# A Fourier filter with routed experts: the 128-point transforms split by a radix-2 step into four tiles of the matrix engine

## The chip, the cores and the metric

One core of one Trainium2 chip runs the kernel. It has five engines with a queue of instructions each: TensorE (PE: matmuls; PEld: its weight loads), VectorE (DVE), ScalarE (ACT), GpSimd (POOL) and SyncE (SP), which only issues transfers; ACT and POOL issue transfers too (rows with a q, as ACTq). An engine works through its own queue in order and waits on semaphores for the others. The time is the device time of one execution in microseconds, the median of the runs.

## The reference

The input x has 8 batches of 3072 rows with 256 features. Each feature is filtered along the rows in the frequency domain, and the result goes through a layer of experts that takes every row at most once.

```python
X = np.fft.rfft(x, axis=1)
Y = X * (filt_r + 1j * filt_i)[None, :, :]
x = np.fft.irfft(Y, n=3072, axis=1).reshape(24576, 256)

logits = x @ w_gate                      # 8 experts, softmax, the largest one is taken
# expert e keeps the first 768 rows that chose it, in order of the rows
h = np.maximum(np.einsum('ecd,edf->ecf', disp, w1), 0.0)   # 768 rows, 1024 wide
y = np.einsum('ecf,efd->ecd', h, w2)
# a kept row becomes gate * y, every other row of the output is zero
```

Since an expert keeps only its first 768 rows, the kernel transforms three batches (FIRST = 3), looks whether every expert is full, and transforms the other five only where one is not. In the runs here three were enough.

## The kernel before

**The transform.** 3072 is split as 128 times 24 (N1 = 128, N2 = 24): row 24*n1 + n2. The steps for batch t are these.

1. `x_load` brings x in six chunks of four n2 (x_in, 128 partitions by n1). `pe_a` multiplies each half chunk by the 128x128 matrix wa, a 128-point Fourier transform over n1 that gives 64 real and imaginary pairs ("units"), into one of two PSUM banks; `act_a` copies it on ScalarE to t_out (three buffers for six chunks; for batch 0 the last three go to v_in) and stores it to DRAM (zt, the profile's t_scratch), two stores a chunk: the even partitions, then the odd ones. Batch 0 goes through this alone; later batches within the stage of the batch before (stage 0 from its step 8, else from step 0, in four steps, A_STEPS).
2. Stage t: `z_load` brings zt back in eight groups, with frequencies of n2 on partitions. In each of 16 steps h `pe_forward` makes eight 64x64 tile matmuls into the PSUM tile wide, VectorE multiplies by the filter (pq, line 599), and in every even step from 2 on, and once after the last, `pe_inverse` makes the inverse transform over n2 of two earlier steps into back; `act_back` copies to v_out and stores to DRAM (vt, u_scratch).
3. Tokens of batch t, within the next stage: `v_load` brings six chunks into v_in (three buffers, each waiting until the matmuls of the chunk three earlier are done), `pe_product` multiplies by the 128x128 matrix wai, `act_rows` copies to y and `act_rows_out` stores the rows (y_rows); `pe_turn` transposes with the identity, `pe_logits` and `pe_raw` make the expert scores. `pe_tokens` and `act_tokens` call them by a step i from 0 to AI_SPAN-1: product i, turn i-1, logits and raw behind. They start at step h = AI_FROM = 4, in the last stage at AI_EARLY = 3, and what is left over runs on in the next stage.
4. Routing of a batch: 30 short VectorE steps (`dve_route`) from the scores to the list of tokens, in the last stage a few per step h (STEPS_BY) behind each pq, later in `dve_last`. Two small matmuls (`pe_rank`, at step ai_from + RANK_STEP) and one set of 24 (`pe_table`) belong to it.

The last batch's tokens have no stage after them: `sp_last`, `pe_last`, `act_last`, `dve_last` and `pool_last` run them alone, beside the routing of batch 1 and the first expert weights (`raw_load` on SP, `act_split` and `low_split`).

**Constants.** wf, wbi and fab (the filter) come in four table groups: group 0 by SP at the start, the others by POOL once batch 0's stores have landed, with batch 1's x between them. Before that fab and wbi are zeroed, by VectorE (wbi, fab's first quarter) and POOL (the rest).

**The experts** follow: 16 blocks of 384 gathered rows, products in two float32 parts, rows scattered to the output. Their code isn't touched.

## Time and profile before

| | |
|---|---|
| time, median of 3 runs | 573.71 us (572.97 to 573.96) |
| the profiled execution: time, span of its instructions | 571.98 us, 570.1 us |
| mean granted TensorE clock | 0.944 of full speed |
| TensorE matmul busy | 483.7 us (85%) |
| VectorE, ScalarE, POOL busy | 220.1, 213.7, 216.8 us |
| moved by DMA | 121.22 MB, mean 213 GB/s |

The span runs from the first to the last instruction. Busy shares are averages over parts of unlike kind: transforms until about 248 us, experts after it. Times in the rows below are microseconds from the start of the span; names in front of an arrow are what an instruction writes.

### The profile page before, as it was taken

What the parts mean: (1) busy time and instruction counts of PE and PEld (TensorE: products, weight loads), DVE (VectorE), ACT (ScalarE), POOL (GpSimd) and SP (SyncE); (2) the same over time, 40 slices, a digit from 0 to 9 for tenths busy, and PEclk for the clock granted to TensorE, in tenths of its full rate; (3) what the DMA queues carried; (4) which work ended last, traced back from release to release, by engine and by line L of the source; (5) the groups of instructions that cost most, each with busy time, mean ns of one, the idle gap of its engine ahead of it and who ended that gap; (6) DMA issues with size and microseconds to landing.
All of it is one profiled execution on the core that took longest, in us unless ns stands there. A gap on an engine that the chain in (4) does not pass through costs nothing.

```text
span 570.1 us, 9642 instructions
## 1 busy us (share of the span) xinstructions
PE 483.7 (85%) x3864; PEld 386.9 (68%) x3864; DVE 220.1 (39%) x334; ACT 213.7 (37%) x378; POOL 216.8 (38%) x189
## 2 busy tenths in 40 slices
PE   5457676899989958977981699999999999999995
PEld 2124232355545534667971699999999999999994
DVE  6024132233355769167700453324433244332210
ACT  2202222444525535635110445424454244443320
POOL 7070100000000000484077227765587655876212
PEclk9859998999989988899986799999999999999999
DMA  8899997979677649789721021983119741193001
GB/s 293 304 348 414 411 309 242 324 246 288 209 243 263 214 133 341 275 291 407 255 83 55 18 93 43 384 296 113 46 62 388 279 129 37 57 389 129 28 21 43
DMA packets 63973, 121.22 MB, mean 213 GB/s; under 512 B 7696, under 2 KB 35120, under 8 KB 63920
## 3 DMA queue, kind: packets, MB, share of 16 engines
q1 hardware_dynamic: 37824, 66.17, 33.4%
q10 hardware_dynamic: 16304, 29.01, 14.3%
q0 software_dynamic: 9792, 25.34, 12.4%
q8 instruction: 33, 0.54, 0.4%
q14 instruction: 20, 0.16, 0.1%
HBM read 60.69 MB, written 59.81 MB: 211 GB/s over the span
## 4 chain that ended last, share of the span: by engine, by line
PE 73%; DMA 8%; issue 5%; DVE 5%; ACT 4%; ACTq 3%; SPq 0%; POOLq 0%; POOL 0%; DVEq 0%
PE back L1050 22%; PE wide L1036 12%; PE bank L1036 12%; PE back L364 7%; PE bank L390 6%; PE wide L351 4%; PE bank L379 3%; DMA v_in<-u_scratch 3%; DMA t_scratch<-t_out 2%; PE bank L403 2%; ACTq L505 2%; DVE pq L599 2%; PE bank L1019 2%; PE bank L417 1%; ACT t_out L498 1%
## 5 line engine op out<-in xcount | busy, mean ns | idle before, releaser
L1050 PE MATMUL back<-w2h,hh 128*128 128x256 f32 x384 | 110.4, 288 | 1.0 <-ACT o_out L823 1.0
L1050 PE MATMUL back<-w2l,hh 128*128 128x256 f32 x384 | 109.3, 285 | 0.0
L1050 PE MATMUL back<-w2h,hl 128*128 128x256 f32 x384 | 109.3, 285 | 0.0
L599 DVE TENSOR_TENSOR pq<-wide,fab 128x1024 f32<-128x1024 f32 x48 | 58.8, 1224 | 118.2 <-PE wide L351 118.2
L865 DVE SCALAR_TENSOR_TENSOR hl<-wide,hh 128x384 fp32r<-128x384 f32 x64 | 34.6, 555 | 133.8 <-ACT hh L814 104.8
L954 POOL DMA_INDIRECT out<-o_out,token x48 | 52.3, 1090 | 82.2 <-ACT o_out L823 72.6
L1050 PEld LDWEIGHTS back<-w2h,hh 128*128 128x128 f32 x384 | 74.3, 194 | 1.2 <-ACT o_out L823 1.2
L1050 PEld LDWEIGHTS back<-w2h,hl 128*128 128x128 f32 x384 | 74.4, 194 | 0.0
L1050 PEld LDWEIGHTS back<-w2l,hh 128*128 128x128 f32 x384 | 74.3, 194 | 0.0
L926 POOL DMA_INDIRECT g_in<-y_rows,token x48 | 51.4, 1072 | 57.2 <-DVE token L737 35.1
L823 ACT ACTIVATE o_out<-back,o_gate 128x256 f32<-128x256 f32 x48 | 22.7, 476 | 103.4 <-PE back L1050 86.5
L1036 PE MATMUL wide<-xh,w1h 128*128 128x384 f32 x128 | 44.6, 349 | 18.9 <-issue 17.0
L379 PE MATMUL bank<-x_in,wa 128*128 128x512 f32 x72 | 40.4, 683 | 18.3 <-ACT t_out L498 11.9
L938 POOL DMA_INDIRECT o_gate<-gate_rows,token x48 | 48.7, 1014 | 14.6 <-issue 14.6
L917 POOL DMA_DIRECT2D gate_rows<-gate x3 | 1.7, 569 | 134.7 <-DVE gate L672 93.8
L364 PE MATMUL back<-pq,wbi 64*48 64x256 f32 x768 | 51.0, 407 | 2.0 <-DVE pq L599 2.0
L351 PE MATMUL wide<-z_in,wf 64*64 64x256 f32 x384 | 33.0, 414 | 21.6 <-DMA z_in<-t_scratch 11.7
L512 ACT COPY v_out<-back 112x1024 f32<-112x1024 f32 x24 | 24.3, 1013 | 59.9 <-PE back L364 53.6
L865 DVE SCALAR_TENSOR_TENSOR hl<-bank,hh 128x384 fp32r<-128x384 f32 x64 | 35.0, 555 | 29.4 <-ACT hh L814 22.4
L390 PE MATMUL bank<-v_in,wai 128*128 128x512 f32 x72 | 41.9, 668 | 4.7 <-DMA v_in<-u_scratch 3.8
L814 ACT ACTIVATE hh<-wide 128x384 fp32r<-128x384 f32 x64 | 30.4, 492 | 40.3 <-PE wide L1036 18.5
L1036 PE MATMUL bank<-xh,w1h 128*128 128x384 f32 x128 | 43.6, 340 | 1.9 <-DVE hl L865 1.9
(109 smaller groups left out, 802.8 us busy)
## 6 DMA issues: line engine op xcount, KB each, us to landing
out<-zero SPq DMA_DIRECT2D x24, 1024.0 KB
w_raw<-in_w SPq DMA_DIRECT2D x16, 1024.0 KB
u_scratch<-v_out ACTq DMA_DIRECT2D x48, 192.0 KB, 3.6
v_in<-u_scratch SPq DMA_DIRECT2D x36, 256.0 KB, 5.2
y_rows<-y ACTq DMA_DIRECT2D x18, 512.0 KB, 3.8
t_scratch<-t_out ACTq DMA_DIRECT2D x30, 256.0 KB, 6.2
z_in<-t_scratch SPq DMA_DIRECT2D x24, 256.0 KB, 3.8
x_in<-in_x POOLq DMA_DIRECT2D x12, 512.0 KB, 15.3
```

The source lines that it names most:

```text
L351: mm = nc.tensor.matmul(wide[out_half, a, 0, :], wf[half, 2 * h + k, :], z_in[half, g % ZB, (2 * h + k) % GP, :], start=True, stop=True)
L364: mm = nc.tensor.matmul(back[part(a), k, s, :], wbi[half, a, 2 * j + s, f, :], pq[half, (2 * n + s) % 3, a, f, :], start=(f == 0), stop=(f ...
L379: nc.tensor.matmul(ps[i % 2][:, :], wa[:, :], x_in[:, c, 2 * h:2 * h + 2, :], start=True, stop=True).then_inc(a_done, 1)
L390: nc.tensor.matmul(ps[i % 2][:, :], wai[:, :], v_in[:, c % 3, 2 * h:2 * h + 2, :], start=True, stop=True).then_inc(ya_done, 1)
L599: nc.vector.tensor_tensor(pq[:, n % 3], wide[:, :, 0, :].unsqueeze(2).to_broadcast([P, 2, 2, D]), fab[:, h], ALU.mult).then_inc(m_done, 1)
L814: nc.scalar.activation(hh[:, b % 2, f, :], ps[(2, 3, 6, 7)[f % 4]][:, 0:TOK], ACT.Relu).then_inc(hh_done, 1)
L865: nc.vector.scalar_tensor_tensor(out=hl[:, b % 2, f, :], in0=ps[(2, 3, 6, 7)[f % 4]][:, 0:TOK], scalar=0.0, in1=hh[:, b % 2, f, :].bitcast ...
L926: nc.gpsimd.indirect_dma_start(out=g_in[:, b % 2, s, :], out_offset=None, in_=yd[0:have], in_offset=bass.IndirectOffsetOnAxis(ap=tokens_of ...
L938: nc.gpsimd.indirect_dma_start(out=o_gate[:, b % 4, s:s + 1], out_offset=None, in_=gd[0:have], in_offset=bass.IndirectOffsetOnAxis(ap=toke ...
L954: nc.gpsimd.indirect_dma_start(out=out, out_offset=bass.IndirectOffsetOnAxis(ap=tokens_of(r, b, s), axis=0), in_=o_out[:, b % 2, s, :], in ...
L1036: mm = nc.tensor.matmul(ps[(2, 3, 6, 7)[f % 4]][:, 0:TOK], wt[:, k, h, f * P:(f + 1) * P], xx[:, b % 2, h, :], start=(m == 0), stop=(m == 5))
L1050: mm = nc.tensor.matmul(ps[4 + (b * ST + s) % 2][:, 0:D], hx[:, b % 2, f, s * P:(s + 1) * P], wt[:, k, f, :], start=(f == 0 and m == 0), s ...
```

## The change

It replaces each 128-point transform by two of 64 points and a sum and difference.

- **First stage.** x now lies in DRAM as [batch, third, partition, half k, 4, 256], so that one `x_load` of 1 MB fills a third of x_in with 8 KB per partition; partition g*64 + n holds rows n and n + 64 (k = 0, 1) of n1, for one of two sets g of twelve n2. `dve_fold` on VectorE makes the sum and the difference of the two halves in place. `pe_a` then takes a chunk in four matmuls with a 64x64 tile of wa each (QUADRANTS), into one of two pairs of banks (low, and high as long as t < 6). `act_a` copies a chunk at once. t has six buffers: t_out and v_in for batches 0 and 1, t_out and y for batch 2. `t_store` stores 64 neighbouring partitions at a time; for batch 0 SP issues it, behind table group 0.
- **Inverse.** `pe_product` takes a chunk in four 64x64 quadrants: one half of the result from the even units, one from the odd. `act_rows` copies the odd part, `dve_rows` on VectorE adds and subtracts it. Rows are stored in two transfers per chunk.
- **Last batch.** `v_load` puts chunks 3 to 5 into z_in's place, which is free by then, and products alternate between low and wide. Chunk 3 is issued ahead of the first weight load, chunks 4 and 5 behind it.
- **Order.** Token steps go by whole chunks (product at even i, turn i-2, logits, raw one later, AI_SPAN 16); RANK_STEP is 2, STEPS_BY differs, A_AT gives the chunks per step. Folds of batch 1 stand behind pq of steps 6, 7 and 8 of stage 0, the first two of batch 2 behind pq of its last two steps, the third in stage 1's step 0. In `dve_last` joins stand behind routing steps 16, 18, 21, 23 and 25, the last behind the tokens. fab is zeroed by POOL alone, SP's first tables wait for one of its four pieces.
- **Routing.** Partitions hold other rows now, so carry and base have two parts per expert, and the gates go out in two stores.

```diff
+NM = N2 // 2 // CH
+QUADRANTS = ((0, 0), (1, 1), (0, 1), (1, 0))
-AI_SPAN = 15
+AI_SPAN = 16
+A_AT = [[0, 1], [2], [3, 4], [5]]
-RANK_STEP = 4
+RANK_STEP = 2
+ROWS_AFTER = [16, 18, 21, 23, 25]
-STEPS_BY = [0, 0, 0, 3, 6, 8, 10, 12, 14, 16, 19, 22, 24, 26, 27, 28]
+STEPS_BY = [0, 0, 0, 3, 7, 9, 12, 14, 16, 18, 20, 22, 24, 26, 27, 28]
...
-            eng.dma_start(x_in[:, c], x[t, :, c * CH:(c + 1) * CH, :]).then_inc((x_first if t in (0, FIRST) else x_loaded)[c], 16)
+            eng.dma_start(x_in[:, m], x[t, m]).then_inc((x_first if t in (0, FIRST) else x_loaded)[m], 16)
...
+        def v_buffer(c, alone):
+            return z_in if alone and c >= 3 else v_in
...
-            if n >= 3:
-                sp.wait_ge(ya_done, (n - 2) * 2)
+            if alone and c >= 3:
+                sp.wait_ge(b_done, (t + 1) * NH)
+            elif n >= 3:
+                sp.wait_ge(ya_done, n - 2)
             sp.nop(nofuse=True)
             for a in range(2):
-                sp.dma_start(v_in[a:P:2, c % 3], vt[t, a].rearrange("(n r) (p d) -> (r p) n d", r=2, d=D)
+                sp.dma_start(v_buffer(c, alone)[half(a), c % 3], vt[t, a].rearrange("(n r) (p d) -> (r p) n d", r=2, d=D)
...
         def sp_last(sp, t, r):
-            for c in range(3):
-                v_load(sp, t, c)
+            for c in range(4):
+                v_load(sp, t, c, True)
             sp.wait_ge(bi_done, (t + 1) * NG)
             raw_load(sp, r, 0, 0)
+            for c in range(4, NCH):
+                v_load(sp, t, c, True)
             raw_load(sp, r, 0, 1)
-            for c in range(3, NCH):
-                v_load(sp, t, c)
...
+        def a_pair(t, c):
+            return high if t < 2 * FIRST and c % 2 else low
+        def pe_a(pe, t, c):
+            both_pairs = t < 2 * FIRST
+            if c % 2 == 0:
+                pe.wait_ge(folded, t * NM + c // 2 + 1)
+            if t * NCH + c >= 2:
+                pe.wait_ge(t_evac, t * NCH + c - (1 if both_pairs and c > 0 else 0))
+            if c < 2 and t >= 2:
+                pe.wait_ge(ya_evac, (t - 2) * NCH)
+            at = 2 * (c % 2)
+            for g, a in QUADRANTS:
+                mm = nc.tensor.matmul(a_pair(t, c)[half(a), g].rearrange("p h d -> p (h d)"), wa[half(g), half(a)],
+                                      x_in[half(g), c // 2, a, at:at + 2, :], start=True, stop=True)
+            mm.then_inc(a_done, 1)
+        def y_pair(c, alone):
+            return wide if alone and c % 2 else low
+        def pe_product(pe, t, c, a_so_far, alone):
...
+            for a, g in QUADRANTS:
+                mm = nc.tensor.matmul(y_pair(c, alone)[half(g), a].rearrange("p h d -> p (h d)"), wai[half(a), half(g)],
+                                      v_buffer(c, alone)[half(a), c % 3, 2 * g:2 * g + 2, :], start=True, stop=True)
+            mm.then_inc(ya_done, 1)
...
+            if 0 <= i < 12 and i % 2 == 0:
+                pe_product(pe, t, i // 2, a_so_far, alone)
+            if 0 <= i - 2 < 12:
+                pe_turn(pe, t, i - 2, alone)
             if 4 <= i and i % 2 == 0:
-                pe_raw(pe, t, (i - 4) // 2)
+                pe_logits(pe, t, (i - 4) // 2, ranked)
+            if 5 <= i and i % 2 == 1:
+                pe_raw(pe, t, (i - 5) // 2)
...
+        def t_buffer(t, c):
+            return t_out if c < 3 or t >= FIRST else y if t == FIRST - 1 else v_in
+        def t_store(eng, t, c):
+            for a in range(2):
+                at = a * 32 + c * 2 * CH if c < 4 else A1 + a * 16 + (c - 4) * 2 * CH
+                dst = zt[t, at:at + 2 * CH].rearrange("(n r) (p d) -> (r p) n d", r=2, d=D)
+                eng.dma_start(dst, t_buffer(t, c)[half(a), c % 3]).then_inc(t_written[c % 3], 16)
+        def act_a(act, t, c):
+            if t > 0 and not (t == FIRST - 1 and c >= 3):
+                act.wait_ge(t_written[c % 3], (t * 2 + (c // 3 if t >= FIRST else 0)) * 32)
+            act.wait_ge(a_done, t * NCH + c + 1)
+            nc.scalar.copy(t_buffer(t, c)[:, c % 3].rearrange("p (g j) d -> p g (j d)", g=2),
+                           a_pair(t, c)[:, :, :, :].rearrange("p g h d -> p g (h d)")).then_inc(t_evac, 1)
+            if t not in (0, FIRST):
+                act.wait_ge(t_evac, t * NCH + c + 1)
+                t_store(act, t, c)
...
+            nc.scalar.copy(y[:, c % 3, 2:4, :], y_pair(c, alone)[:, 1]).then_inc(odd_out, 1)
...
+        def dve_fold(dve, t, m):
...
+            first, second = (x_in[:, m, k].rearrange("p f d -> p (f d)") for k in range(2))
+            nc.vector.tensor_tensor(first, first, second, ALU.add).then_inc(sums_set, 1)
+            dve.wait_ge(sums_set, t * NM + m + 1)
+            nc.vector.scalar_tensor_tensor(out=second, in0=second, scalar=-2.0, in1=first,
+                                           op0=ALU.mult, op1=ALU.add).then_inc(folded, 1)
+        def dve_rows(dve, t, c, alone):
+            dve.wait_ge(odd_out, t * NCH + c + 1)
+            even, first, second = y_pair(c, alone)[:, 0], y[:, c % 3, 0:2, :], y[:, c % 3, 2:4, :]
+            nc.vector.tensor_tensor(first, even, second, ALU.add).then_inc(e_added, 1)
+            nc.vector.tensor_tensor(second, even, second, ALU.subtract).then_inc(ya_evac, 1)
...
+                if a is not None and 0 <= h + 2 - a_from < NM:
+                    dve_fold(dve, a, h + 2 - a_from)
+                if nxt is not None and h >= NH - 2:
+                    dve_fold(dve, nxt, h - (NH - 2))
+                if ai is not None and 0 <= h - ai_from < 12 and (h - ai_from) % 2 == 0:
+                    dve_rows(dve, ai, (h - ai_from) // 2, False)
...
-                sp.wait_ge(fab_clear, 2 * r + 2)
+                sp.wait_ge(fab_clear, 4 * r + 1)
+                sp.wait_ge(wbi_clear, r + 1)
                 sp.nop(nofuse=True)
                 load_tables(sp, 0)
+                for c in range(NCH):
+                    sp.wait_ge(t_evac, first * NCH + c + 1)
+                    sp.nop(nofuse=True)
+                    t_store(sp, first, c)
```

## Rows read from the trace of the kernel before

**Rows 1.** Chain of waits, 0 to 250 us: start, length, what.

```profile
1.20 4.00 DMA x_in<-in_x
...
27.69 4.23 DMA z_in<-t_scratch
...
50.34 0.47 PE wide L351 x8
...
52.20 0.66 PE wide L351 x8
...
61.46 13.55 DMA t_scratch<-t_out
...
113.91 1.10 PE bank L390 x2
...
137.47 0.44 PE bank L403 x4
...
153.68 1.02 ACT v_out L512
...
206.03 1.02 ACT v_out L512
...
219.53 9.28 DMA v_in<-u_scratch
...
248.14 2.00 PE wide L1036 x10
```

**Rows 2.** Timeline of TensorE at 90.8 us: start, length, instruction, [idle before <-releaser].

```profile
90.82 0.66 PE L351 MATMUL wide<-z_in,wf 64*64 64x256 f32 x8 [1.39 <-DMA z_in<-t_scratch]
```

**Rows 3.** Windows of 5 us: busy time by engine, granted clock, DMA share, GB/s.

```profile
40.00:45.00 5.00, 3.57 (x48) 2.12 (x44) 1.75 (x2) 1.01 (x1) 0.00 (x0) 0.81 1.02 407
...
85.00:90.00 5.00, 3.10 (x56) 1.56 (x47) 1.50 (x2) 1.45 (x2) 0.00 (x0) 1.00 0.60 188
```

**Rows 4.** Windows of token steps: PE, PEld, DVE, ACT, POOL busy, clock, DMA, GB/s.

```profile
113.90:153.60 39.70, 39.69 (x474) 22.35 (x476) 13.98 (x12) 19.61 (x34) 0.00 (x0) 1.00 0.77 248
163.70:206.00 42.30, 41.68 (x494) 23.48 (x498) 28.49 (x42) 20.62 (x36) 0.56 (x1) 1.00 0.67 225
```

**Rows 5.** Groups of instructions by line: busy us, mean ns of one, idle before.

```profile
L599 DVE TENSOR_TENSOR pq<-wide,fab 128x1024 f32<-128x1024 f32 x48 | 58.8, 1224 | 118.2 <-PE wide L351 118.2
...
L512 ACT COPY v_out<-back 112x1024 f32<-112x1024 f32 x24 | 24.3, 1013 | 59.9 <-PE back L364 53.6 <-DMA u_scratch<-v_out 4.1 <-issue 2.1
...
L860 DVE TENSOR_TENSOR xl<-bank,xh 128x384 fp32r<-128x384 f32 x32 | 16.6, 550 | 13.3 <-issue 10.9 <-ACT xh L806 2.5
...
L1210 POOL MEMSET fab<- 128x4096 f32 x3 | 10.4, 3512 | 0.3 <-POOLq L1249 0.3
```

**Rows 6.** Timeline of ScalarE in stage 1's first steps.

```profile
95.36 1.07 ACT L498 COPY t_out<-bank 128x512 f32<-128x512 f32 x2 [4.79 <-issue]
96.46 1.25 ACTq L505 DMA_DIRECT2D t_scratch<-t_out  x2
```

**Rows 7.** Loads of batch 1's x, issued 33 to 37 us: ns per issue, landing.

```profile
L285 POOL DMA_DIRECT2D x_in<-in_x x6: 550/558/562, 33.8 to 36.4; - x6
...
DMA to landing us min/median/max: 16.0/19.9/23.3
```

**Rows 8.** Timeline of VectorE: the end of batch 1's routing, its tokens.

```profile
225.64 1.36 DVE L715 TENSOR_TENSOR hot_hi<-hot_eq,nums 128x1152 bf16<-128x1152 bf16 x1
...
234.09 0.21 DVE L737 SCALAR_TENSOR_TENSOR token<-t_sum 128x48 uint32<-128x48 f32 x1
```

**Rows 9.** DMA queues, 40 to 50 us: packets, MB, share of 16 engines.

```profile
q0 software_dynamic: 819, 2.97, 74.2%
...
q10 hardware_dynamic: 126, 0.39, 9.8%
```

**Rows 10.** DMA share in 40 slices, 203.3 to 206.5 us: one v_out pair.

```profile
DMA  0000000000793999089853697937395210000000
```

**Rows 11.** DMA share in 40 slices, 113.8 to 117 us: from slice 16, one t_out pair.

```profile
DMA  8999999988432112899999999999999999610000
```

More of the change, by code:

```diff
@@ L916, in gate_store @@
             pool.nop(nofuse=True)
-            pool.dma_start(gd.rearrange("(b p n) one -> b p (n one)", p=P, n=N2)[t], gate[:, :]).then_inc(gate_stored, 16)
+            for g in range(2):
+                pool.dma_start(gd.rearrange("(b k n g c) one -> b g n k (c one)", b=B, k=2, n=A1, g=2)[t, g],
+                               gate[half(g), :].rearrange("p (k c) -> p k c", k=2)).then_inc(gate_stored, 16)
         def pool_gather(pool, r, b):
@@ L1138, in run @@
             def run(r, first, last):
-                for i in range(12):
-                    pe_a(pe, first, i)
+                for c in range(NCH):
+                    pe_a(pe, first, c)
                 stages(first, last, lambda t, a, a_from, ai, ai_from, before, rt: pe_stage(
@@ L1154, in run @@
             def run(r, first, last):
-                for i in range(12):
-                    act_a(act, first, i)
+                for c in range(NCH):
+                    act_a(act, first, c)
                 if r == 0:
@@ L1193, in run @@
             def run(r, first, last):
-                stages(first, last, lambda t, a, a_from, ai, ai_from, before, rt: dve_stage(dve, t, r, rt, t > first + 2))
+                if r > 0:
+                    for m in range(2):
+                        dve_fold(dve, first + 1, m)
+                stages(first, last, lambda t, a, a_from, ai, ai_from, before, rt: dve_stage(
+                    dve, t, r, a, a_from, t + 2 if t + 2 < last else None, ai, ai_from, rt, t > first + 2))
                 dve_last(dve, last - 1, r)
@@ L1217, in run @@
                 load_tables(pool, 2)
-                for c in range(NCH):
-                    x_load(pool, first + 1, c)
+                for m in range(NM):
+                    x_load(pool, first + 1, m)
                 load_tables(pool, 3)
@@ L1223, in stage @@
                     if a is not None and a + 1 < last:
[L1224 to L1225 removed]
+                        for m in range(NM):
+                            x_load(pool, a + 1, m)
                     if rt is not None:
@@ L1253 @@
     i = _np.arange(P)
-    squares = _np.stack([_np.eye(P), i[:, None] < i[None, :], _np.ones((P, P))], 1).astype(_np.float32)
     per = _np.zeros((P, 3, E * N2), _np.float32)
     per[:, 0] = _np.tile(_np.arange(E), N2)
-    per[:, 1] = _np.tile(_np.arange(N2) > 0, E)
+    per[:, 1] = _np.tile(_np.arange(N2) % (N2 // 2) > 0, E)
     per[:, 2] = _np.repeat(_np.arange(E) * CAP, N2)
-    token = N2 * i[:, None] + _np.arange(N2)
+    n = _np.arange(N2)
+    token = N2 * (i[:, None] % A1 + n // 12 * A1) + 12 * (i[:, None] // A1) + n % 12
+    turn = 2 * (i % A1) + i // A1
+    squares = _np.stack([_np.eye(P), turn[:, None] < turn[None, :], _np.ones((P, P))], 1).astype(_np.float32)
     numbers = _np.concatenate([_np.tile(_np.arange(1, P + 1), (P, 1)), _np.tile(_np.arange(NHI), (P, 1)),
```

244 lines of the change are left out of this document (116 added, 128 removed).

## The prediction

> **What bounds the kernel now.** The page's busy shares come first: TensorE is busy most of the time, but everything after 248 us is the experts' matmuls, which the diff leaves alone. Only the first 248 us can move, and an average over them prices nothing, so I cut them by the chain of waits [rows 1] into seven stretches.
>
> (1) Batch 0's first transform, until its last t_scratch store has landed and the read of z_in starts at 27.69. (2) Stage 0, until stage 1's first forward matmul at 90.82 [rows 2]. In it the chain stands 13.55 us on t_scratch stores, since t_out has three buffers for six chunks, and the window at 40 us says why a store is slow there: a full DMA share, 407 GB/s [rows 3]. (3) Stage 1's first four steps, until the first inverse product at 113.91: ScalarE copies and issues in turn. (4) Stage 1's token steps, until the v_out copy at 153.68: TensorE 39.69 of 39.70 us busy [rows 4], so a pair of steps costs 6.62, a sixth. (5) v to DRAM and back, until 163.70. (6) Stage 2, until the v_out copy at 206.03: TensorE again, 41.68 of 42.30, VectorE 28.49 [rows 4]. (7) Batch 2's tokens alone, until the experts' first matmul at 248.14, with 9.28 us on one v_in chunk, which waited for a buffer and stood behind two 1 MB weight loads.
>
> **Prices.** Per chunk a transform goes from two 128x512 matmuls to four 64x64 quadrants of 512 columns. An old matmul (two records) takes 1.10 on the path. Eight records of 64x256 take 0.47 when more follow, 0.66 when TensorE starts anew [rows 1]; twice the columns are bounded by 0.9 and 1.3. I take 1.1, nearest to the old matmul with as many columns: one matmul per chunk is saved.
>
> VectorE gets new work. A fold is two 128x1024 instructions; pq has that size and takes 1.224 [rows 5]: 2.4 a fold, three per batch. Joining a chunk's halves (add, subtract, 128x512) lies between xl at 384 columns, 0.550, and pq at 1024: 0.685 each by the straight line, less what two in a row overlap; 1.3 the two, 7.8 per batch. ScalarE's work per chunk falls in the first stage from a pair of copies at 1.07 [rows 6] to one of 1.01 (as v_out, 1.013 [rows 5]), in the inverse to half a pair; its store issues stay at 1.25 per chunk [rows 6].
>
> **The sum** (in brackets the total so far).
>
> (1) x's first half megabyte came at 5.2 [rows 1]; at 0.4 MB/us thirds land near 6.5, 9.1 and 11.6. Folds end at 9.0, 11.6 and 14.1; six quadrant sets at a cold 1.8 and copies at 1.01 end near 20.5, 2 us early. But the stores move from ScalarE's queue to SP's, past table group 0 (2.1 MB). SP's queue is in order: x done 11.6, tables 16.8, then 3.1 MB of stores, each pair 0.52 MB in 1.6 (20 of 40 slices of 3.2 us [rows 11]): landed 26.4. The read starts 0.6 earlier [-0.6]. Bounds: -2.3 with queues that share freely, +4.5 if a pair takes 2.45 (below). POOL's fourth memset (3.5 [rows 5]) ends near 15 and is hidden by the wait for the stores; without that cover it would cost its length.
>
> (2) Six buffers (t_out and v_in) remove the 13.55. Late next is VectorE's queue: batch 1's folds stand at steps 6 to 8, in front of the pq behind them, and wait for x. Its chunks were issued at 33.8 to 36.4 and landed 16.0 to 23.3 later [rows 7], so thirds land at 50.5, 55.0 and 59.1. Step 6's pq ends at 49.2; then fold to 52.9, pq, fold to 57.4, pq, fold to 61.5. TensorE, and with it ScalarE and the inverses, queue behind that. Then nothing waits for a buffer: a step is 1.86 (50.34 to 52.20 [rows 1]), plus inverses and transforms, and step 15 with batch 2's first two folds ends at 81. Batch 1's stores are issued by 69. The DMA then has moved or must move 20 MB since 27: at 0.41 MB/us that is 76, and z's 4.2 make 80. The later one sets it: first forward at 81.7 [-9.1]. Bounds: 0 if the last store lands no earlier than before, -13.5 if the stall were simply cut out.
>
> (3) ScalarE's first copy to the product, 95.36 to 113.91, was 18.6. Now six copies at 1.01, five issues at 1.25, one v_out copy and store 1.9: 14.3, -4.3 [-13.4].
>
> (4) One matmul less is 1.1 per pair, 6.6 in all, if TensorE stays the limit. It doesn't. AI_FROM is even, so product, logits and inverse share the even step; in the odd one only turn (0.44) and raw (some 0.15) stand between its forward and the next, which waits for pq: 1.86 from forward to forward, of which forward, turn and raw fill 1.1. A pair is 6.62 - 1.1 + 0.75 = 6.27, six give -2.0, and the last inverse has nothing left in front of it to cover pq: +1.4. -0.6 [-14.0]. Bounds: -6.6 and 0.
>
> (5) The same chain: 0.
>
> (6) AI_EARLY is odd, the steps balance, and VectorE decides: 28.49 busy and 7.8 of joins: 36.3, in order. Idle: 1.9 until the first odd half is copied; about 2.5 around the rank matmul, which RANK_STEP 2 puts in the same step as the scan that it reads, so that TensorE stands in front of it with everything behind; 1.6 for later odd halves; the last inverse, 1.9. That is 44.2 against 42.3: +1.9 [-12.1]. Bounds: -6.6 with VectorE hidden, +5 with double idle.
>
> (7) The 9.28 goes. Late next is VectorE again: batch 1's routing ended at 227.0, and the tokens came at 234.3 [rows 8], of which some 4 were lost to that same wait. Now it starts 1.7 later (token step 16: one more copy, logits and raw before the table), carries five joins (6.5) and waits some 2.8 for their odd halves, less the 4: tokens 7.0 later, and behind them on VectorE expert 0's split, on POOL the gathers, on SP expert 1's weights. Some 3 of it are covered, since the gathers landed ahead of the last token matmuls: +4 [-8.1]. Bounds: -9.3 and +8.
>
> At nothing: the second y store issue per chunk, at most 0.65 (half of 1.25) on ScalarE, busy 19.61 of 39.70 [rows 4], 3.9 per batch without that cover; POOL's second gate store; one short carry step per batch.
>
> The profiled execution lasted 571.98 (span 570.1); 571.98 - 8.1 = 563.9. It stands 1.7 under the median of the runs, 573.71, so I say **565.6**.
>
> **The new partitions.** t's stores and v's loads move from every second partition to 64 neighbouring ones; now only v_out's stores use neighbours. In the saturated window their 0.39 MB, 96 packets of 4 KB, took 9.8% of 16 engines for 10 us, 0.163 us each, and x's 2.97 MB, 725 packets, took 74.2%, 0.164 [rows 9]: no dearer. Alone, a v_out pair (0.39 MB) is in motion for 23 of 40 slices of 3.2 us [rows 10], 212 GB/s, where t_out's makes 325 [rows 11]; but its slices are only some two thirds busy, so its issue slowed it more than the engines. The sum prices the layout at nothing; 212 GB/s (2.45 for a pair) is the bound.
 The saturated rows do not bear it out, and the lone pair neither proves nor excludes it.
>
> **Rivals.** *Slow halves*: a store pair takes 2.45. (1) then ends at 31.5, 5.1 later than forecast, and the first v chunks of (5) and (7) come 0.85 later each: 565.6 + 6.8 = 572.4. For it the lone pair, against it the saturated packets. Chance 0.2.
> *DMA floor*, slower: stage 0 moves the same bytes, and if the engines spend the 13.55 on batch 2's x, now issued earlier, ahead of batch 1's stores, z returns no sooner. Place: batch 1's last t_scratch store; price: the 8.5 of (2), and 2 for the folds in front of stage 1's pq: 576. It decides from that store landing at 86. For it: the full share at 40; against: 0.60 at 85 to 90 [rows 3]. Chance 0.2.
> *VectorE keeps up*: the idle times of (6) and (7) fit into gaps; (6) gains 4 and (7) loses nothing: 565.6 - 5.9 - 4 = 556. For it: 28.49 of 42.30 busy; against: the order of its queue. Chance 0.17.
> *Nothing moves*: each gain is met by a VectorE wait, 573.7. Chance 0.06.
>
> Forecast 0.37, 560 to 570. Faster: 0.37, 0.17 and two thirds of the slow halves, 0.68; slower 0.2; same 0.12 (within 0.2%, about what a measurement of this kernel can tell from no change). The range, 553 to 576, leaves out the far half of the DMA floor and the outer ends of the other cases.
>
> **What would show it.** After: no t_scratch wait in stage 0; stage 1's first forward near 82, its first product near 100; pairs of 6.3 with TensorE waiting for pq; stage 2 at 44 with VectorE the releaser; in the last tokens no v_in wait, but joins late on VectorE; experts from 240. Wrong, if a lone t_scratch pair takes over 2 us, if batch 1's last store lands after 86, or if stage 2 is under 40.

## The result, and the profile after

The changed kernel takes 590.77 us (median of 4, 589.37 to 593.61) against 573.84 for the kernel before on the same chip: ratio 1.0301, 95% interval 1.0258 to 1.0344. It is 3% slower; forecast were 565.6 and a range of 553 to 576. The profiled execution of after lasted 589.37, 17.4 more than that of before. Cut at the places that the prediction used (differences of the cut times; the prediction's 27.69 is the second transfer of z, so the table takes the second in both, at 26.60 in after; the first was issued at 27.16 and 26.05):

| stretch | before | forecast | after |
|---|---|---|---|
| (1) until the read of z_in | 27.69 | 27.1 | 26.60 |
| (2) from there to stage 1's first forward | 63.13 | 54.6 | 64.29 |
| (3) to the first product | 23.09 | 18.8 | 22.89 |
| (4) to the v_out copy | 39.77 | 39.2 | 40.34 |
| (5) to the next product | 10.02 | 10.0 | 10.09 |
| (6) to the last v_out copy | 42.33 | 44.2 | 46.94 |
| (7) to the experts' first matmul | 42.11 | 46.1 | 52.97 |
| the rest of the span | 322.0 | 322.0 | 323.4 |

Steps (1), (4) and (5) came within 1.2 us. Steps (2) and (3) gave none of the 12.8 that they were to give, and (6) and (7) cost 9.6 more than forecast.

Stage 0's end in the windows of after (start and end, length, busy us of PE, PEld, DVE, ACT and POOL, granted clock, DMA share, GB/s):

```profile
75.00:80.00 5.00, 3.95 (x40) 2.30 (x40) 0.00 (x0) 1.92 (x2) 0.00 (x0) 0.50 1.04 392
80.00:85.00 5.00, 3.39 (x56) 1.92 (x48) 3.51 (x3) 1.51 (x2) 0.00 (x0) 0.94 0.78 252
85.00:90.00 5.00, 2.48 (x24) 1.35 (x28) 4.79 (x5) 0.51 (x1) 0.00 (x0) 0.74 0.84 254
```

The DMA is full until 80, as it was in the kernel before at 40 [rows 3], and VectorE is busy 4.79 of the last 5 us. What happens there, in the tile view of t_scratch, between 78.5 and 86:

```profile
L311 SPq DMA_DIRECT2D z_in<-t_scratch x4: 457/569/597, 84.1 to 85.9; - x4
L532 ACTq DMA_DIRECT2D t_scratch<-v_in x2: 597/1137/1677, 78.1 to 78.8; - x2
...
DMA to landing us min/median/max: 2.7/4.4/5.2
```

Batch 1's last store is issued at 78.8 (forecast 69) and lands 5.2 later, at 84.0 (forecast 76); the read of z follows at 84.1. In the kernel before it landed at 86.6. So 2.6 us were won. They were lost again at once, in VectorE's and TensorE's timelines (start, duration, instruction, in brackets the idle time before it and its releaser):

```profile
83.86 1.22 DVE L636 TENSOR_TENSOR x_in<-x_in 128x1024 f32<-128x1024 f32 x1
85.11 1.23 DVE L638 SCALAR_TENSOR_TENSOR x_in<-x_in 128x1024 f32<-128x1024 f32 x1
86.25 1.22 DVE L656 TENSOR_TENSOR pq<-wide,fab 128x1024 f32<-128x1024 f32 x1
87.38 1.22 DVE L636 TENSOR_TENSOR x_in<-x_in 128x1024 f32<-128x1024 f32 x1
88.63 1.23 DVE L638 SCALAR_TENSOR_TENSOR x_in<-x_in 128x1024 f32<-128x1024 f32 x1
```

```profile
87.52 3.54 PE L385 MATMUL back<-pq,wbi 64*48 64x256 f32 x32 [2.71 <-DVE pq L656]
90.89 0.60 PE L372 MATMUL wide<-z_in,wf 64*64 64x256 f32 x8
```

Step 15's pq stood behind a fold of batch 2 (83.86 to 86.3), TensorE waited 2.71 us, the granted clock fell (0.74 on average over the window), and the inverse took 3.54 instead of some 1.95. Stage 1's first forward came at 90.89, against 90.82 [rows 2]. The prediction had these folds in front of step 15 too, and let them set the start of stage 1, but at 81.

The stages that follow, in the windows of after (columns as above), which answer to [rows 4]:

```profile
113.80:154.10 40.30, 35.27 (x480) 20.25 (x480) 21.20 (x23) 16.14 (x26) 0.00 (x0) 0.95 0.80 236
164.20:211.20 47.00, 38.40 (x506) 21.41 (x507) 36.49 (x56) 17.46 (x31) 1.22 (x2) 0.96 0.73 210
211.20:264.10 52.90, 33.56 (x286) 20.32 (x285) 33.45 (x59) 19.97 (x33) 12.35 (x8) 0.68 0.74 206
```

In stage 1 TensorE is no longer full (35.27 of 40.30): it waits for pq, with a pair of steps at 6.43 where 6.27 was forecast. In stage 2 VectorE is busy 36.49, where 36.3 was forecast; but its idle time is 10.5 and not 7.9. The stage loses most at its start, in TensorE's timeline:

```profile
169.66 0.66 PE L372 MATMUL wide<-z_in,wf 64*64 64x256 f32 x8 [1.97 <-DVE pq L656]
174.03 0.40 PE L478 MATMUL high<-lg,sq 128*128 128x16 f32 x2 [2.27 <-DVE lg L730]
175.76 3.35 PE L385 MATMUL back<-pq,wbi 64*48 64x256 f32 x32
```

1.97 us in front of a forward (pq behind a join and three routing steps), 2.27 in front of the rank matmul, and behind that wait an inverse of 3.35 (granted clock 0.57 on average from 176 to 180).

The last tokens, in ScalarE's timeline of after:

```profile
236.56 0.58 ACT L563 COPY y<-wide 128x512 f32<-128x512 f32 x1 [2.40 <-DMA y_rows<-y]
...
240.65 1.90 ACT L849 CAST w2h<-w_raw 128x2048 fp32r<-128x2048 f32 x1 [2.39 <-DMA w_raw<-in_w]
```

The wait of 9.28 us on a v chunk is gone. In its place ScalarE waits for a y buffer whose store has not landed, and then for expert 0's second weight. What VectorE waits for in front of the tokens, in its timeline (a table step of the routing, then two joins):

```profile
217.77 0.25 DVE L794 TENSOR_TENSOR table<-table,back 128x96 f32<-128x96 f32 x1 [6.04 <-PE back L485]
...
237.18 0.69 DVE L645 TENSOR_TENSOR y<-wide,y 128x512 f32<-128x512 f32 x1 [3.26 <-ACT y L563]
...
243.55 0.69 DVE L645 TENSOR_TENSOR y<-low,y 128x512 f32<-128x512 f32 x1 [2.55 <-ACT y L563]
```

The tokens came 39.4 us after the last v_out copy, where before it was 28.1. The table step waits 6.04 instead of 3.50 (+2.5), five joins take 6.5, their waits for odd halves 6.8 (the two above and one of 0.97), and a wait of 3.97 for the second table is gone: together 11.8, where the tokens came 11.3 later. In the whole stretch TensorE was busy 33.6 us instead of 30.8, at a granted clock of 0.69 instead of 0.84.

### The profile page after: what moved, and what is told of

It reads as the page before. It is cut to its first block, busy times and chain, and to the rows that moved or that the text cites. A ratio compares the mean times of both kernels' runs of the same rounds, so it can differ in the third digit from the quotient of the medians.

```text
span 587.5 us, 9953 instructions
## 1 busy us (share of the span) xinstructions
PE 466.5 (79%) x4008; PEld 382.2 (65%) x4008; DVE 262.8 (45%) x390; ACT 203.4 (35%) x342; POOL 219.2 (37%) x187
## 4 chain that ended last, share of the span: by engine, by line
PE 60%; DVE 10%; issue 9%; ACTq 6%; DMA 6%; ACT 6%; SPq 1%; POOL 1%; POOLq 0%; DVEq 0%
PE back L1125 21%; PE wide L1111 12%; PE high L1111 11%; PE back L385 6%; DMA x_in<-in_x 4%; DVE pq L656 3%; ACTq L532 3%; PE low L1094 2%; PE wide L372 2%; ACT v_out L549 2%; PE low L423 1%; SPq L532 1%; DMA y_rows<-y 1%; ACTq L554 1%; ACT t_out L538 1%
## 5 line engine op out<-in xcount | busy, mean ns | idle before, releaser
L1001 POOL DMA_INDIRECT g_in<-y_rows,token x48 | 51.5, 1073 | 65.7 <-DVE token L810 43.6
L372 PE MATMUL wide<-z_in,wf 64*64 64x256 f32 x384 | 34.2, 426 | 37.9 <-DVE pq L656 23.5
L385 PE MATMUL back<-pq,wbi 64*48 64x256 f32 x768 | 54.9, 431 | 8.0 <-ACT v_out L549 4.1
L1111 PE MATMUL wide<-xh,w1h 128*128 128x384 f32 x128 | 45.9, 358 | 18.2 <-issue 12.7
L991 POOL DMA_DIRECT2D gate_rows<-gate x6 | 3.7, 618 | 150.1 <-DVE base L746 105.5
L385 PEld LDWEIGHTS back<-pq,wbi 64*48 64x48 f32 x768 | 30.8, 137 | 28.6 <-issue 15.6
L938 DVE SCALAR_TENSOR_TENSOR hl<-high,hh 128x384 fp32r<-128x384 f32 x64 | 35.2, 555 | 31.6 <-ACT hh L887 23.7
L372 PEld LDWEIGHTS wide<-z_in,wf 64*64 64x64 f32 x384 | 14.0, 145 | 53.9 <-issue 28.4
L1111 PE MATMUL high<-xh,w1h 128*128 128x384 f32 x128 | 43.9, 343 | 2.7 <-DVE hl L938 2.7
L1111 PE MATMUL wide<-xh,w1l 128*128 128x384 f32 x128 | 45.1, 352 | 0.0
```

Source lines behind the costliest of these rows:

```text
L372: mm = nc.tensor.matmul(wide[out_half, a, 0, :], wf[half, 2 * h + k, :], z_in[half, g % ZB, (2 * h + k) % GP, :], start=True, stop=True)
L385: mm = nc.tensor.matmul(back[part(a), k, s, :], wbi[half, a, 2 * j + s, f, :], pq[half, (2 * n + s) % 3, a, f, :], start=(f == 0), stop=(f ...
L938: nc.vector.scalar_tensor_tensor(out=hl[:, b % 2, f, :], in0=ps[(2, 3, 6, 7)[f % 4]][:, 0:TOK], scalar=0.0, in1=hh[:, b % 2, f, :].bitcast ...
L1001: nc.gpsimd.indirect_dma_start(out=g_in[:, b % 2, s, :], out_offset=None, in_=yd[0:have], in_offset=bass.IndirectOffsetOnAxis(ap=tokens_of ...
L1111: mm = nc.tensor.matmul(ps[(2, 3, 6, 7)[f % 4]][:, 0:TOK], wt[:, k, h, f * P:(f + 1) * P], xx[:, b % 2, h, :], start=(m == 0), stop=(m == 5))
```

## The experiments

Each kernel was timed in turns with the kernel before on its chip, which took 571.7 to 575.5 us there, and 555.7 on one chip, where three of them ran (joins on GpSimd, and two edits of the kernel before); so ratios are compared, and stretches that lie before the experts. The changed kernel's ratio is 1.0301. Among kernels that leave a stretch as the changed kernel has it, stage 1 started between 87.6 and 92.0 us and its first product came between 111.2 and 115.1; stage 2 took 46.9 to 48.7, the last tokens 51.5 to 53.8. Within these ranges a single profile settles nothing.

**Stage 0: who holds back the stores.** First, batch 1's stores on SyncE (edits are shown in short):

```
 act_a:     if t not in (0, 1, FIRST): ... t_store(act, t, c)
 sp_stage:  + after z_load(0, 7): for c in range(NCH): wait t_evac; t_store(sp, 1, c)
```

> Batch 1's twelve t_scratch stores are issued from SyncE's queue, which is idle from 62 us on, instead of from ScalarE's. Theory (ScalarE is the chain of stage 0 after the folds: it stands 1.3 to 2.8 us in each chunk's issues while the DMA is full, and with it the inverses): the last store lands 3 us or more before 84.0, batch 1's z follows, and stage 1's first forward comes near 88, bounded there by batch 2's folds: about -3 us, 588. Rival (DMA floor: the same bytes are in the queues whoever issues them): the last store still lands within 1 us of 84.0, stage 1's first forward stays within 1 us of 90.9, and the time stays within 1 us of 590.8.

Ratio 1.0339 (1.0279 to 1.0399). TensorE's timeline:

```profile
80.68 3.08 PE L390 MATMUL back<-pq,wbi 64*48 64x256 f32 x32 [3.50 <-ACT v_out L554]
92.86 1.13 PE L377 MATMUL wide<-z_in,wf 64*64 64x256 f32 x8 [9.10 <-DMA z_in<-t_scratch]
```

Freed of the issues, stage 0's arithmetic is over before 84, and TensorE then stands 9.1 us for z: the theory about ScalarE falls. The last store landed at 87.6, with 22.14 MB moved after 27 us, so the rival's 84 was not met either: on SyncE's queue single issues took up to 3.99 us and the last was made at 80.9. Why they took longer there was not tried.

Then batch 2's folds two steps earlier (`NH - 4 <= h < NH - 2`):

> Batch 2's first two folds stand behind steps 12 and 13 of stage 0 instead of 14 and 15, where VectorE stood idle 7.3 us in the changed kernel. Theory (the folds in front of step 15's pq, and behind it the last inverse, decide when stage 1 starts, while z landed near 88.4): stage 1's first forward comes near 88.5 instead of 90.89, -2.4 us, 588.4. Rival (z, that is the DMA, sets it, or x of batch 2 is not there yet at step 12): first forward still at 90 or later, time within 1 us of 590.8.

First forward at 90.45, ratio 1.0303 (1.022 to 1.0386): no gain shows. The last store landed at 84.5, so z was no earlier, and 90.45 is within the range of that start. The folds of batches 1 and 2 without their time:

```
-  first, second = (x_in[:, m, k].rearrange("p f d -> p (f d)") for k in range(2))
+  first, second = (x_in[:, m, k].rearrange("p f d -> p (f d)")[:, 0:CH * D if t in (0, FIRST) else 16] for k in range(2))
```

> The folds of batches 1 and 2 keep their place and their waits for x, but work on 16 columns instead of 1024, so that the rest of x is not folded; VectorE loses 2.4 us per fold. Theory (stage 0 is at the DMA floor, so the folds cost only what stands in front of stage 0's last inverse): batch 1's last store lands within 1.5 us of 84, stage 1's first forward comes near 88.5, its first product near 111: -2 to -3 us. Rival (the folds in VectorE's queue are what makes stage 0 long): stage 1's first forward at 86 or earlier, -5 us.

The last store landed at 83.8, the first forward came at 87.84, the product at 110.34, ratio 1.0281 (1.0197 to 1.0366). Without the folds' time the stores land where they did, as the theory said. That some 3 us return behind them is likely but not shown: 87.84 also occurs with the folds, the product is 0.8 earlier than in any kernel with them, and the ratios overlap.

Last, x of batch 2 behind batch 1's stores:

```
 stage (GpSimd): + for i in range(3): pool.wait_ge(t_written[i], (a + 1) * 64)
                   for m in range(NM): x_load(pool, a + 1, m)
 dve_stage:        fold m of batch 2 behind stage 1's pq of step m
```

> Batch 2's x is loaded only when batch 1's last t_scratch store has landed, and its three folds stand behind stage 1's first three pq. Theory (stage 0 is at a DMA floor, and batch 2's 3.1 MB of x, which now come early, stand in front of batch 1's stores): the last store lands 5 us or more before 84.0, stage 1's first forward comes near 84 instead of 87.6 to 92.9, and some 5 us are given back in stage 1's first steps, where the three folds stand in front of pq: about 588. Rival (the stores are late because ScalarE issues them late): the last store lands within 2 us of 84, the forward stays at 87 or later, and the folds make it slower, 594.

The last store landed at 78.0, the first forward came at 84.63, the product at 112.13 (the folds gave back 4.6, as expected), ratio 1.0247 (1.0188 to 1.0307). The late x was then tried in the kernel before, which has no folds, with six buffers for batch 1:

> The kernel before with two edits: batch 1's first stage has six buffers (t_out and v_in), and batch 2's x is loaded only when batch 1's last t_scratch store has landed. Theory (stage 0 is at a DMA floor set by what is loaded ahead of batch 1's stores; six buffers give nothing without that): the last store lands near 79 instead of 86.6, stage 1's first forward comes at 84 instead of 90.8, and batch 2's transforms then wait 1 to 3 us for their x: -4 to -5 us against the kernel before. Rival (what is taken out of stage 0 is all given back in stage 1's first steps, which then wait for x): within 1.5 us of the kernel before.

Ratio 0.9922 (0.9885 to 0.9958), first forward at 84.53, but first product at 113.92: in the trace all of it was given back, at one place, in ScalarE's timeline:

```profile
102.14 1.07 ACT L498 COPY t_out<-bank 128x512 f32<-128x512 f32 x2 [7.61 <-DMA t_scratch<-t_out]
```

Batch 2's first stage had three buffers still. So the next kernel gives it six (chunks 3 to 5 in y, as the changed kernel does), and a second one has the twelve buffers without the late x:

```
 act_a:  buf = (v_in if t in (0, 1) else y if t == FIRST - 1 else t_out) if c >= 3 else t_out
```

> The kernel before with batch 2's x after batch 1's stores (as in the run on stage 0 before) and six first-stage buffers for batch 2 as well (its chunks 3 to 5 in y). Theory (that run started stage 1 6.3 us earlier and gave all of it back at one place, 7.6 us in which ScalarE waited for t_out's third-last store): the first product comes near 107 instead of 113.9, the experts start 5 to 6 us earlier: ratio 0.983 to 0.990. Rival (the DMA share of 1.03 after 85 us makes the stores of batch 2 late for something else, such as v's loads): the first product at 112 or later, ratio 0.992 or more.

> The kernel before with the changed kernel's six first-stage buffers alone, for batches 1 and 2, and batch 2's x as early as its buffers allow. By the prediction's second step this part was worth 8.5 us in stage 0. Theory (stage 0 is at the DMA floor): the waits on t_scratch go, the last store of batch 1 lands within 3 us of 86.6, stage 1's first forward comes no more than 3 us earlier; stage 1's first steps lose their short waits for a buffer (1 to 3 us): ratio 0.99 to 1.0. Rival (the prediction): first forward at 84 or earlier, ratio 0.985.

With the late x: ratio 0.9888 (0.9834 to 0.9942; 565.09 against 572.53), last store landed at 76.6, first forward 83.51, first product 106.75, experts 242.68. Buffers alone: 0.9946 (0.9911 to 0.9981), last store 83.2, first forward 87.35, product 110.71. Both beat both kernels; their intervals overlap, so the late x alone shows in the stretches (store 6.6 us earlier, product 4.0) and not in the time. What the DMA moved from 27 us until batch 1's last store had landed, in the DMA views of before, after and the late x:

```profile
DMA packets 8602, 21.37 MB, mean 359 GB/s; under 512 B 1067, under 2 KB 4187, under 8 KB 8598
```

```profile
DMA packets 7723, 21.34 MB, mean 374 GB/s; under 512 B 964, under 2 KB 4084, under 8 KB 6952
```

```profile
DMA packets 7627, 17.88 MB, mean 360 GB/s; under 512 B 944, under 2 KB 4064, under 8 KB 7623
```

The same 21.4 MB in both kernels (21.36 with the buffers alone, at 379 GB/s). With 3.5 MB fewer ahead of it, the store lands 6.6 us earlier than with the buffers alone, in a kernel that differs in nothing else: these bytes hold it back. They are not all of it. In the kernel before the DMA share was 0.82 from 75 to 80 and 0.94 to 85, and the last store was issued only at 81.1, behind the buffers' waits; the buffers alone won 3.4 us.

**The layout.** Stores of t and loads of v over every second partition (`half(a)` becomes `a:P:2` in both):

> The t_scratch stores and the v loads use every second partition, as in the kernel before, instead of 64 neighbours; the rows then come to the wrong partitions, so this kernel computes a transform of permuted rows with the same work. Theory (64 neighbouring partitions move more slowly when nothing else fills the engines: the lone pair near 115 us takes some 2.9 us instead of 1.6, and v_in's loads near 220 us ran at 225 GB/s at full share instead of 270): a lone pair takes 1.6 again, the v loads of the last tokens run at 270 GB/s or more, and the time falls by 4 to 8 us. Rival (the layout costs nothing, and the rates differ because of what else is in the queues): rates as in the changed kernel, time within 1.5 us of 590.8.

Ratio 1.0174 (1.0105 to 1.0243), an interval apart from the changed kernel's, but from another chip: on this one the kernels of the runs on y's stores and the v chunks' place, below, stand at 1.0261 and 1.0242, their times 3 us longer. The lone pair after 113 us, in the DMA views of after and of this kernel from 107 to 119 (busy tenths and GB/s in 40 slices of 0.3 us):

```profile
DMA  9999999999999999999999995278998997000000
GB/s 389 382 382 376 382 382 386 386 379 389 369 369 396 406 434 372 386 376 386 372 389 417 427 396 205 109 195 201 205 167 171 300 324 236 24 20 0 0 0 0
```

```profile
DMA  9999998899999788523899991000000000097289
GB/s 369 328 335 372 416 382 290 300 345 341 379 355 365 195 246 314 219 82 72 294 331 324 341 324 34 24 24 24 10 0 0 0 0 0 0 164 96 82 314 382
```

Behind a first weak slice the pair is in motion with neighbours for eight slices (195 to 236, mean 225 GB/s, 2.4 us), with every second partition for five (294 to 324, mean 323, 1.5 us); the two bounds that the prediction had were 212 and 325. While v's loads fill the DMA in the last tokens, from some 4.6 us after the first of them was issued, first in after and then in this kernel:

```profile
220.00:225.00 5.00, 3.14 (x16) 1.73 (x20) 4.22 (x14) 0.07 (x1) 1.17 (x2) 0.50 1.13 227
```

```profile
217.00:222.00 5.00, 4.60 (x20) 1.73 (x20) 4.29 (x14) 0.58 (x1) 1.17 (x2) 0.50 0.93 277
```

227 GB/s at a share of 1.13 against 277 at 0.93. The first three chunks of these loads had landed 10.3 us after the first issue in after and 8.6 in this kernel; in all twenty traces it is 9.4 to 10.8 with neighbours and 8.1 to 8.9 with every second partition. The last tokens took 50.65 instead of 52.97. The theory holds for the rates; in time the layout is worth some 3 to 7 us, by the chip with which one compares. Stage 0's start gave nothing: the first read of z came at 26.40, against 26.05. The Trainium skill (SBUF — State Buffer, "Door 1: The DMA port swizzle") says that such a half reaches 8 of 16 ports; an estimate by its figure per port, 27.2 GB/s, is 218. This case's runs agree (225 and 227).

**Stage 2.** The rank matmul one step later (RANK_STEP 3, routing steps as before):

> The rank matmul moves one step later than the scan that it reads (RANK_STEP 3), and the routing steps stand as in the kernel before. Theory (in stage 2 TensorE stood 2.27 us in front of the rank matmul, fell to the lower clock and paid the next inverse at 3.35 instead of 1.95): stage 2 from its first inverse product to its last v_out copy falls from 46.9 to about 43.5, -3.4 us, 587.4. Rival (VectorE's 36 us of work in order are the bound, so that the wait only moves to the next pq): stage 2 within 1 us of 46.9, time within 1 us of 590.8.

Stage 2 took 48.05, ratio 1.0358 (1.0301 to 1.0416), no gain: TensorE waited 4.3 us for pq and 2.7 at the logits. Batch 1's y stores on SyncE:

> Batch 1's y_rows stores in stage 2 are issued from SyncE's queue instead of ScalarE's. Theory (ScalarE's order sets stage 2's pair of 6.55: inverse, v_out copy, its two issues, odd half, two y issues, y_t, lg_t, raw, inverse): without 1.25 of issues per pair stage 2 falls from 46.9 to 48.0 in the runs so far to about 43, 587. Rival (VectorE's work in order is the bound): stage 2 stays at 46 or more, and the time within 1.5 us of 590.8.

45.88, ratio 1.0261 (1.0205 to 1.0316): 1 us, between theory and rival. The joins on GpSimd:

> The joins of the inverse's halves go from VectorE to GpSimd, which stands idle in these stages; since it is given SBUF only here, ScalarE copies both halves of a chunk (1.01 instead of 0.59) and GpSimd adds, scales and adds in place. Only the last chunk of the last batch stays on VectorE. Theory (VectorE's queue, with 7.8 us of joins per batch in front of pq and of the routing, is what makes stage 2 and the last tokens long): stage 2 falls from 46.9 to 43 or less, and the last tokens from 53 to 49 or less: 583. Rival (the engines' order behind each other decides, so a join that takes three GpSimd instructions is late for the turns whoever does it): both stretches within 1.5 us of the changed kernel, or longer; 590 or more.

47.59 and 56.4, ratio 1.0321 (1.0261 to 1.0381). VectorE had time, and the pair still took up to 7.7: a join took GpSimd three instructions of 1.27, 1.49 and 1.27 (VectorE: 0.69 and 0.68), and TensorE's products waited for them (in stage 2, total, times, longest):

```profile
PE low L424 <- POOL y L659: 5.4, 4, 3.0
```

So this run doesn't price VectorE's time. The next one does:

```
-  even, first, second = y_pair(c, alone)[:, 0], y[:, c % 3, 0:2, :], y[:, c % 3, 2:4, :]
+  even, first, second = y_pair(c, alone)[:, 0, :, 0:8], y[:, c % 3, 0:2, 0:8], y[:, c % 3, 2:4, 0:8]
```

> The joins of the inverse's halves keep their place, their waits and their semaphores, but work on 16 columns instead of 512, so that the rest of each chunk's sums is left out; VectorE loses some 1.2 us per chunk and nothing else changes. Theory (VectorE's time is what makes stage 2 and the last tokens long, and GpSimd's slower joins hid that): stage 2 falls from 46.9 to 43 or less, the last tokens from 53 to 48 or less: 581. Rival (the order decides: the routing starts a step later, the rank matmul earlier, ScalarE issues more stores): stage 2 falls by no more than 2, the last tokens by no more than 2: 587 or more.

Ratio 1.0178 (1.0111 to 1.0245), stage 2 at 43.12, the last tokens at 50.95:

```profile
166.38:209.50 43.12, 36.60 (x506) 20.38 (x507) 29.94 (x56) 17.07 (x30) 1.23 (x2) 1.00 0.79 224
```

The theory holds for stage 2 (3.8 of the 4.6 us that it grew) and for at most a fifth of the last tokens' growth of 10.9, though VectorE had 6.1 us less to do there (27.33 busy instead of 33.45). Batch 0's tokens a step earlier:

> The changed kernel with batch 0's tokens one step earlier in stage 1 (AI_FROM 3 instead of 4). Then product and inverse stand in different steps of stage 1, and batch 0's logits are done one step earlier in stage 2, where the routing begins. Theory (in stage 1 TensorE waits for pq because the even step holds everything; in stage 2 the long third interval of 11.4 between v_out copies comes from a routing that starts one step later than in the kernel before, with the joins in front of it, while the rank matmul stands earlier): stage 1's pair falls from 6.43 to 5.9 or less, the third interval of stage 2 from 11.4 to 9 or less, together -4 us or more, 586. Rival (ScalarE's order of copies and issues sets the pair wherever the product stands): pairs of 6.4 in stage 1 and an interval over 11 in stage 2, time within 1.5 us of the changed kernel.

Ratio 1.0334 (1.0243 to 1.0426), nothing gained. (Its profiled execution was 6.7 us longer than its median, so its stretches are not read.)

**The last tokens.** The second weight behind chunk 0's y rows (one `wait_ge(y_stored[0], ...)` on SyncE, the copies at steps 9 and 13 instead of 6 and 10):

> In batch 2's last tokens all six v chunks are loaded first, expert 0's second weight load waits until chunk 0's y rows have landed, and ScalarE's copies of that weight and of expert 1's first come three steps later. Theory (the weight loads stand in front of the y_rows stores, so that y's three buffers come free late, 2.4 us at chunk 3, and ScalarE then waits 2.39 us for the weight in front of chunk 4; both pass on to the joins on VectorE and to the tokens): the tokens come at 245 instead of 250.7, the experts' first matmul at 259 instead of 264.1, -5 us, 585.8. Rival (VectorE's joins between the routing steps are the cost): the waits go but the tokens come no more than 1.5 us earlier, 589.5 or more.

Tokens 38.1 after the last v_out copy instead of 39.4, the stretch 50.93 instead of 52.97, ratio 1.0293 (1.0238 to 1.0349): at most 2 us in the stretch, which the time does not show (the rest of the span took 326.7 instead of 323.4). The v chunks back in v_in, with everything else of the change:

> The last batch's v chunks 3 to 5 go to v_in as its buffers come free, behind both of expert 0's weight loads, as in the kernel before; everything else is the changed kernel. By the prediction this part alone removed the wait of 9.28 us, so undoing it would cost 5 or more: 595 or later. Theory (all six chunks and the weights loaded at once fill the DMA, y's stores stand behind them and y's three buffers come free late): the wait on a v chunk comes back, but the one on y_rows goes, and the last tokens stay within 3 us of 53: 588 to 593.

52.83 instead of 52.97, ratio 1.0242 (1.0158 to 1.0327): undoing this part costs nothing. The same part alone in the kernel before:

> The kernel before with only the last v chunks 3 to 5 in z_in's place, loaded in the changed kernel's order. The prediction's price: the wait of 9.28 us on a v chunk goes, the experts start 5 to 9 us earlier, -5 or more. Theory (loading all six chunks and two weights at once fills the DMA; y's stores and the weights then come late, and ScalarE's queue stands at the weight's copy or at a y buffer): the v wait goes and 2 to 4 us of it come back as these waits: -2 to -5. Rival (nothing of the wait is on the path): within 1 us of the kernel before.

Ratio 1.0043 (0.9997 to 1.0088), the stretch 42.91 against 42.11. The tokens came 4.4 us earlier, and ScalarE lost it:

```profile
232.87 1.90 ACT L785 CAST w2h<-w_raw 128x2048 fp32r<-128x2048 f32 x1 [4.79 <-DMA w_raw<-in_w]
```

SyncE had issued that weight at 219.3, behind six v chunks and the first weight; it landed 13.5 us later (ScalarE itself stood 4.79 of them), and the y copies stood behind it in ScalarE's queue. With this copy moved back to step 11 and that of expert 1's weight to step 13, on top of the first edits of stage 0 (late x, six buffers for batch 1 alone):

> The kernel before, with six first-stage buffers for batch 1, batch 2's x after batch 1's stores, the last v chunks in z_in's place, and ScalarE's copies of the second and third weight behind the last tokens' work (steps 11 and 13 instead of 6 and 10). Theory (with the v chunks in z_in's place the 9.28 us came back as 13.5 us in which ScalarE stood in front of the second weight; with that copy later the last tokens shrink): the experts start 3 us or more earlier, counted from stage 2's last v_out copy (42.1 before): ratio 0.985. Rival (the last weights are then late themselves, and the experts wait for them): the last tokens at 42 or more, ratio 0.992 as with the stage 0 edits alone.

The last tokens took 43.0, ratio 1.0016 (0.997 to 1.0061): the rival. The edit made the wait itself, in TensorE's timeline:

```profile
249.44 0.66 PE L1045 MATMUL wide<-xh,w1h 128*128 128x384 f32 x1 [5.17 <-DVE xl L869]
```

On VectorE xl stood behind the split of expert 1's weight (3.41 from 244.95), whose copy now came at 243.0. So this run doesn't tell what the v chunks' place would give with copies that hold up neither the tokens nor the experts. Four edits together in the changed kernel:

> The changed kernel with four edits together: AI_FROM 3, batch 2's x after batch 1's stores, the second weight load behind chunk 0's y rows with ScalarE's copies of weights later, and batch 1's y stores on SyncE. Theory (the costs found one by one lie in different stretches and add up): some 3 us from stage 0 and 1, 3 from stage 2 and its token steps, 3 from the last tokens: ratio to the kernel before 1.01 to 1.015, instead of 1.030. Rival (each wait that is taken out uncovers the next): 1.02 or more.

Ratio 1.0239 (1.015 to 1.0329). The first forward came at 85.64 and the product at 114.14 all the same; stage 2 took 46.7, the last tokens 51.6. The rival: taking out one wait uncovers the next.

## Why the prediction was wrong

Between the forecast for the profiled execution, 563.9, and its 589.4 lie 25.5 us: (2) makes 9.7 of them, (7) 6.9, (3) 4.1, (6) 2.7, (4) 1.1, the rest of the span 1.4; (1) came 0.5 earlier than forecast.

**Step (2), the main error.** "Moved or must move 20 MB since 27: at 0.41 MB/us that is 76": it was 21.3 MB, and 374 GB/s on average, not 410: 84.0. A floor was in the sum; its size was wrong by 8 us. "Batch 1's stores are issued by 69" failed with it: the last was issued at 78.8, since ScalarE stood in its issues (up to 1.99 us each, 0.58 to 0.67 with the late x) and for stores that had not landed. The prediction let six buffers remove the chain's 13.55 us. They are the time in which one t_out store landed; ScalarE stood 4.45 and 6.23 us there, with the DMA full (a share of 1.03 to 1.06 from 60 to 75). Six buffers won 3.4 us of the landing in the kernel before, and here it came 2.6 earlier; the rest of the wait moved to z. The rival "DMA floor" named this place and priced it at 576; its point of decision, 86, was not reached (84.0), and the folds took the rest.

**Step (3).** Six copies and five issues: 15.5 from the first copy to the product where 14.3 was forecast, and 18.6 before. But ScalarE came to the first copy 3 us later: its copy behind stage 0's last inverse was 1.6 late (91.19 against 89.56), and the issues of five constants took 4.85 us, against 3.74 before.

**Steps (1) and (4)** were right: the read 1.1 earlier (forecast 0.6), a pair bound by pq.

**Step (6).** VectorE's work was right to 0.2 us, its idle time 2.6 short. Around the rank matmul it stood 3.4 where 2.5 was forecast (0.88 and 2.53, the second behind the inverse of 3.35), for odd halves 4.0 and not 3.5, and 1.65 in front of two later pq, which the sum did not have; the last inverse cost less. Without the joins' time the stage is 43.1.

**Step (7).** "The 9.28 goes": it went, and a new wait took its place, for y's stores and the weights behind loads that now come all at once. The prediction priced the v chunks' place as a gain and no load as a cost: its waits for odd halves were 2.8 and are 6.8, its later start 1.7 and is 2.5, and of the 3 us that were to be covered behind the tokens only 0.5 were. Alone this part is worth nothing in either kernel, with the copies where they were.

**The new partitions.** The sum took nothing, argued from packets in a saturated window. The lone pair [rows 10, 11] was the better witness than [rows 9]; its 2.4 us after the change are over the 2 that the prediction named as a sign of being wrong. 1.0301 against 1.0174 is 1.3% or some 7 us, on one chip 3 to 4; the rival said 6.8. That 7 and 6.8 agree is luck: the rival put 5.1 of them into (1), which was to end at 31.5, and there the layout cost nothing.

So the rivals were not alternatives. The floor came true near its price in (2), the slow halves as a rate but not at their place, where the forecast gave each 0.2 as if the other were absent; the order of VectorE's and ScalarE's queues took the rest. The single causes tried here (joins 4 to 6 us, folds up to 3, halves 3 to 7, the order of weights up to 2) make at most 18 where 17 were lost, but the run with four edits shows that such prices don't simply add; how the 17 divide stays open.

## What to carry to other kernels

Before a wait for a buffer is taken out, look at the DMA share while the engine waits: if it is full, count the bytes that must go ahead of the last store, since they hold it back more than the buffers do (here 3.5 MB were worth 6.6 us, the buffers 3.4). Then change the order of the loads first (here x behind the stores, with the buffers: 0.9888) and the arithmetic last. Work saved on TensorE is paid back where the new helper work stands in another engine's queue ahead of TensorE's next operand.

## What the hardware showed that was not expected

A DMA issue on ScalarE is no fixed price: the same constant's issue took 0.50 us with the late x in the kernel before, 0.65 before, 2.42 after and 4.66 in the changed kernel with the late x. At a DMA share of 1.13 v's loads moved 227 GB/s over 64 neighbouring partitions, and 277 at 0.93 over every second: the share says that the engines are occupied, not that they move what they could. A weight's load that followed many loads in SyncE's queue took 13.5 us to land, where 1 MB at the 407 GB/s of [rows 3] would be 2.6 (an estimate). GpSimd took 1.27 us to add 128x512, VectorE 0.69.
